# A convolution and two feed-forward layers on one core: the first tile's own tokens loaded apart, the tail's lower rows a step ahead, the last chunk in halves

## The reference

```python
w = exp(weight_gen - max); w /= sum + 1e-9        # [2, 4096, 8 heads, 7 taps]
x_pad = 6 zero tokens in front of each batch, then x    # [2, 4096, 192]
out[b, s, h, :] = sum over k of w[b, s, h, k] * x_pad[b, s + k, h, :]   # 24 channels a head
x = out.reshape(8192, 192)
x = (relu(x @ moe_w_in) ** 2) @ moe_w_out               # 192 -> 2048 -> 192
h = x @ moe2_w_in
out = (h * cos(h)) @ moe2_w_out                         # 192 -> 2048 -> 192
```

## Time and profile before

| | us |
|---|---|
| median of three executions | 1201.99 |
| the profiled execution | 1201.13 |
| its span in the profile | 1199.3 |
| TensorE busy | 1174.4 (98%) |
| VectorE busy | 963.7 (80%) |
| ScalarE busy | 816.2 (68%) |
| GpSimd busy | 369.3 (31%) |

### The profile page before, as it was taken

One profiled execution on the slowest core, in us unless ns is written; L12 is line 12 of the kernel. 1 busy time (PEld: TensorE's weight loads), 2 busy tenths in 40 slices (PEclk: granted clock), 3 DMA queues, 4 the chain that ended last, 5 costly groups with the idle time before them and its releaser, 6 DMA issues.

```text
span 1199.3 us, 25462 instructions
## 1 busy us (share of the span) xinstructions
PE 1174.4 (98%) x9784; PEld 1108.5 (92%) x9784; DVE 963.7 (80%) x1500; ACT 816.2 (68%) x1488; POOL 369.3 (31%) x265
## 2 busy tenths in 40 slices
PE   5999999999999999999999999999999999999997
PEld 4778999899999999999999999999999999999986
DVE  7867888877878787787878878787787878878786
ACT  3887666666666676666666666666666767666675
POOL 3895707052150704307060240705215070000000
PEclk9999999999999999999999999999999999999999
DMA  7432111011110111111011111101111000100000
GB/s 183 103 86 48 34 28 34 8 21 34 28 34 14 18 35 24 34 27 34 12 18 34 28 34 21 35 13 22 34 28 34 13 17 4 25 1 14 1 15 14
DMA packets 112984, 37.30 MB, mean 31 GB/s; under 512 B 101600, under 2 KB 110816, under 8 KB 112864
## 3 DMA queue, kind: packets, MB, share of 16 engines
q1 hardware_dynamic: 110974, 34.75, 13.9%
q10 hardware_dynamic: 1890, 0.93, 0.4%
HBM read 23.84 MB, written 6.29 MB: 25 GB/s over the span
## 4 chain that ended last, share of the span: by engine, by line
PE 87%; DVE 6%; ACT 4%; issue 1%; DMA 0%; SPq 0%; POOL 0%; ACTq 0%; DVEq 0%; POOLq 0%
PE y L557 45%; PE h L557 41%; DVE h L1237 1%; DVE h L1259 1%; DVE turns L1241 1%; ACT turns L1001 1%; DVE g_lo L1272 1%; ACT relu L974 1%; ACT g_hi L1014 1%; DMA xc<-in_x_dram 0%; DVE g_lo L1268 0%; DVE x L1227 0%; ACT arena L957 0%; DVE stat L1129 0%; DVE stat L1120 0%
## 5 line engine op out<-in xcount | busy, mean ns | idle before, releaser
L557 PE MATMUL y<-g_hi,wo 64*128 64x512 f32 x3054 | 703.6, 395 | 1.1 <-DVE g_lo L1163 0.5
L557 PE MATMUL y<-g_lo,wo 64*128 64x512 f32 x2036 | 528.3, 391 | 0.0
L557 PEld LDWEIGHTS y<-g_hi,wo 64*128 64x128 f32 x3054 | 425.2, 184 | 25.0 <-DVE xa_lo L1286 2.8
L478 POOL TENSOR_TENSOR tap<-xc,gen 128x768 f32<-128x768 f32 x98 | 150.9, 1546 | 581.6 <-DVE xd_lo L1249 566.1
L557 PEld LDWEIGHTS y<-g_lo,wo 64*128 64x128 f32 x2036 | 311.7, 184 | 5.1
L557 PE MATMUL h<-xa_hi,wa_hi 64*128 64x512 f32 x1018 | 278.5, 404 | 6.0 <-DVE g_lo L1268 4.1
L1001 ACT ACTIVATE turns<-turns 128x512 f32<-128x512 f32 x238 | 150.4, 632 | 196.8 <-DVE turns L1241 195.8
L557 PE MATMUL h<-xa_hi,wa_lo 64*128 64x512 f32 x1018 | 269.6, 391 | 0.0
L557 PE MATMUL h<-xa_lo,wa_hi 64*128 64x512 f32 x1018 | 269.0, 391 | 0.0
L1259 DVE TENSOR_TENSOR h<-h,turns 128x512 f32<-128x512 f32 x238 | 165.9, 697 | 122.6 <-ACT turns L1001 121.7
L1237 DVE SCALAR_TENSOR_TENSOR h<-h,relu 128x512 f32<-128x512 f32 x249 | 173.4, 696 | 66.9 <-ACT relu L974 64.3
(11 more groups left out here) (101 smaller groups left out, 1092.3 us busy)
## 6 DMA issues: line engine op xcount, KB each, us to landing
xc<-in_x_dram SPq DMA_DIRECT2D x60, 240.0 KB
out_dram<-arena SPq DMA_DIRECT2D x62, 64.0 KB, 1.9
xt_a<-x_blocks SPq DMA_DIRECT2D x224, 16.0 KB, 1.8
arena<-in_moe_w_out_dram SPq DMA_DIRECT2D x16, 192.0 KB, 3.4
arena<-in_moe_w_in_dram SPq DMA_DIRECT2D x16, 128.0 KB, 2.7
out_dram<-arena SPq DMA_DIRECT2D x62, 32.0 KB, 1.7
xt_d<-x_blocks SPq DMA_DIRECT2D x112, 16.0 KB, 1.8
arena<-in_moe_w_in_dram SPq DMA_DIRECT2D x16, 64.0 KB, 3.0
```

The lines of the kernel that those rows point to most:

```text
L478: pool.tensor_tensor(tap[:, k % 2, :].rearrange("p (r g) -> p r g", g=GROUP), rows[k], wk, ALU.mult).then_inc(pool_step, 1)
L557: return pe.matmul(o, w[rows, :], x[rows, :], start=start, stop=stop)
```

## The change

At the start, xc is filled by 11 transfers. `load_first_own` loads the four own rows of each partition in four transfers with a semaphore of their own, `x_own`; `load_first_halo` loads the six halo rows in seven. SP issues seven of the eleven, ScalarE four. The convolution takes the taps from the newest to the oldest: the first product waits for `x_own` only, the second for all. The last product is cut into heads 0 to 5 and heads 6 to 7, the last two sums into channels 0 to 127 and 128 to 191, and TensorE turns part 0 as soon as the first group of channels is complete. One group of eight identity transposes is gone.

In the tail, a slot starts with BOTTOM's first up matmul, ahead of the wait for g_lo, and with the previous chunk's `up_d_top`; BOTTOM's up matmuls are one step ahead of TOP's down matmuls through the slot. Chunk 255's columns go in two halves of 256 from engine to engine, with a bank of h each, and the last three chunks' down matmuls start with the three that need only g_hi, without waiting for g_lo.

```diff
-    FIRST_X = 16 * 8
+    FIRST_OWN = 16 * QUARTERS
+    FIRST_X = 16 * 7
@@ start of SP; ScalarE has the rest
-            load_first_rows(sp, ((0, 0), (0, 1), (0, B), (1, 0)))
+            load_first_own(sp, (0, 1))
+            load_first_halo(sp, ((1, B), (0, 0), (0, 1), (1, 0), (1, 1)))
@@
+        def parts(m):
+            count = 2 if m == STEPS - 1 else 1
+            return [(k, slice(k * TOK // count, (k + 1) * TOK // count)) for k in range(count)]
+        def load_first_own(eng, quarters):
+            for q in quarters:
+                eng.dma_start(xc[q * BLOCK:(q + 1) * BLOCK, HALO * DM:],
+                              x_v[:, q * JJ * DM:(q + 1) * JJ * DM]).then_inc(x_own, 16)
@@ TensorE: the last down matmuls
+            def last_down(k, y, l, f, hi, lo):
+                w = wo[l]
+                for part, cols in parts(k):
+                    part_a, part_d = y[:, 0, cols], y[:, 1, cols]
+                    pe.wait_ge(g2_hi_ready, k + 1 + part)
+                    pe.matmul(part_a, w[:, f, 0:DA], hi[:, cols], start=False, stop=False)
+                    pe.matmul(part_a, w[:, f, 2 * P:2 * DM], hi[:, cols], start=False, stop=False)
+                    pe.matmul(part_d, w[:, f, DA:2 * P], hi[:, cols], start=False, stop=False)
...
@@ TensorE: tail_slot
+                    if m == STEPS - 1:
+                        last_tail_up(m, k)
+                        return
+                    up_a(o, 1, f, of, BOTTOM, 0, start=True)
+                if STEPS - SLOTS < m < STEPS:
+                    end_of_tail_up(m - 1)
+                if m < STEPS:
+                    pe.wait_ge(g2_ready, k + 1)
...
-                for j in range(3):
-                    last = down_a(down, TOP, j, start=j == 0)
-                    up_a(o, 1, f, of, BOTTOM, j, start=j == 0)
-                last.then_inc(tail_a_left, 1)
-                pe.wait_ge(down2_done, k)
-
-                top = m >= STEPS - SLOTS
-                down_d(down, TOP, 0, start=True)
+                for j in range(2):
+                    up_a(o, 1, f, of, BOTTOM, j + 1)
+                    down_a(down, TOP, j, start=j == 0)
                 up_d(o, 1, f, of, 0)
-                down_d(down, TOP, 1).then_inc(tail_d_left, 1)
+                down_a(down, TOP, 2).then_inc(tail_a_left, 1)
                 if not top:
                     up_d(o, 1, f, of, 1)
                 up_d(o, 1, f, of, 2).then_inc(h2_left, 1)
+                pe.wait_ge(down2_done, k)
+                down_d(down, TOP, 0, start=True)
                 pe.wait_ge(tail_a_left, turn)
                 down_a(down, BOTTOM, 0)
+                down_d(down, TOP, 1).then_inc(tail_d_left, 1)
                 down_a(down, BOTTOM, 1)
+                down_a(down, BOTTOM, 2, stop=True).then_inc(tail_a_done, 1)
                 pe.wait_ge(h2_left, m)
                 up_a(o, 1, f, of, TOP, 0)
-                down_a(down, BOTTOM, 2, stop=True).then_inc(tail_a_done, 1)
-                up_a(o, 1, f, of, TOP, 1)
                 pe.wait_ge(tail_d_left, turn)
                 down_d(down, BOTTOM, 0)
+                up_a(o, 1, f, of, TOP, 1)
+                down_d(down, BOTTOM, 1, stop=True).then_inc(down2_done, 1)
                 last = up_a(o, 1, f, of, TOP, 2, stop=not top)
@@ TensorE: start
-            for k in range(TAPS - 1):
+            for k in range(TAPS - 2):
...
             pe.wait_ge(first_sum, TAPS - 1)
+            turn_x1(0, 0)
+            pe.wait_ge(first_sum, TAPS + 1)
             pe.wait_ge(pad_zeroed, 1)
-            for part in range(2):
-                turn_x1(0, part)
+            turn_x1(0, 1)
@@ ScalarE: tail_chunk (VectorE's in the same way)
                 if m < STEPS:
-                    act.wait_ge(up2_done, m + 1)
                     act.wait_ge(g2_made, m - 1)
-                    act.activation(turns[:, c, :], h[:, tail_bank(m), :], ACT.Copy,
-                                   bias=0.25).then_inc(turns_ready, 1)
+                    for part, cols in parts(m):
+                        act.wait_ge(up2_done, m + 1 + part)
+                        act.activation(turns[:, c, cols], h[:, tail_bank(m + part), cols], ACT.Copy,
+                                       bias=0.25).then_inc(turns_ready, 1)
```

More of the change, by code:

```diff
@@ L665, in downs_of_slot, with end_of_tail_up, last_tail_up @@
                         pe.wait_ge(piece_ready[PL + (m - D2) // PF], 3)
+            def end_of_tail_up(m):
+                f = m % SLOTS
+                if f % 4 == 0:
+                    pe.wait_ge(w_copied, f // 4 + 1)
+                    pe.wait_ge(x2_hi_ready, 2 * TILES + 1)
+                up_d_top(h[:, tail_bank(m), :], f, stop=True).then_inc(up2_done, 1)
+            def last_tail_up(m, k):
+                f, of = m % SLOTS, m // SLOTS % 2
+                (o, cols), (o2, cols2) = [(h[:, tail_bank(m + part), :], at) for part, at in parts(m)]
+                down = (y1, 1, k % SLOTS, g2_hi[:, k % 2, :], g2_lo[:, k % 2, :])
+                turn = k - (TAIL - LAG - TAIL_D2) + 1
+                up_a(o, 1, f, of, BOTTOM, 0, cols, start=True)
+                up_a(o, 1, f, of, BOTTOM, 1, cols)
+                end_of_tail_up(m - 1)
+                up_a(o, 1, f, of, BOTTOM, 2, cols)
+                up_d(o, 1, f, of, 0, cols)
+                pe.wait_ge(g2_ready, k + 1)
+                pe.wait_ge(tail_a_done, turn - 1)
+                down_a(down, TOP, 0)
+                up_d(o, 1, f, of, 2, cols).then_inc(h2_left, 1)
+                pe.wait_ge(g2_ready, m - 2)
+                up_a(o2, 1, f, of, BOTTOM, 0, cols2, start=True)
+                down_a(down, TOP, 1)
+                up_a(o2, 1, f, of, BOTTOM, 1, cols2)
+                up_a(o2, 1, f, of, BOTTOM, 2, cols2)
+                down_a(down, TOP, 2).then_inc(tail_a_left, 1)
+                up_d(o2, 1, f, of, 0, cols2)
+                up_d(o2, 1, f, of, 2, cols2).then_inc(h2_left, 1)
+                pe.wait_ge(down2_done, k)
+                down_d(down, TOP, 0)
+                pe.wait_ge(h2_left, m)
+                up_a(o, 1, f, of, TOP, 0, cols)
+                up_a(o, 1, f, of, TOP, 1, cols)
+                pe.wait_ge(tail_a_left, turn)
+                down_a(down, BOTTOM, 0)
+                up_a(o, 1, f, of, TOP, 2, cols)
+                up_d_top(o, f, cols, stop=True).then_inc(up2_done, 1)
+                down_a(down, BOTTOM, 1)
+                down_d(down, TOP, 1).then_inc(tail_d_left, 1)
+                down_a(down, BOTTOM, 2).then_inc(tail_a_done, 1)
+                pe.wait_ge(h2_left, m + 1)
+                up_a(o2, 1, f, of, TOP, 0, cols2)
+                up_a(o2, 1, f, of, TOP, 1, cols2)
+                pe.wait_ge(tail_d_left, turn)
+                down_d(down, BOTTOM, 0)
+                up_a(o2, 1, f, of, TOP, 2, cols2)
+                up_d_top(o2, f, cols2, stop=True).then_inc(up2_done, 1)
+                down_d(down, BOTTOM, 1).then_inc(down2_done, 1)
@@ L685, in tail_slot @@
                 if m >= STEPS:
-                    pe.wait_ge(down2_done, k)
-                    down_alone(*down).then_inc(down2_done, 1)
+                    if m == STEPS:
+                        pe.wait_ge(down2_done, k)
+                    last_down(k, *down)
                     return
@@ L716, in tail_slot @@
                     last.then_inc(up2_done, 1)
[L717 to L722, removed]
             def last_downs(m, o, f, of):
@@ L1208, in convolve_first @@
                 total = x1[:, 0:JJ * DM]
+                last = TAPS - 1
+                wide = -(-DA // GROUP)
                 def product(k):
@@ L1228, in convolve_first @@
                                       ALU.add).then_inc(first_sum, 1)
+                last_product(0, wide)
+                dve.wait_ge(first_product, last)
+                dve.wait_ge(first_sum, last - 2)
+                channel_sum(last - 1, 0, DA)
+                last_product(wide, HEADS)
+                dve.wait_ge(first_product, last + 1)
+                dve.wait_ge(first_sum, last - 1)
+                channel_sum(last, 0, DA)
+                channel_sum(last - 1, DA, DM)
+                dve.wait_ge(first_product, last + 2)
+                dve.wait_ge(first_sum, last + 1)
+                channel_sum(last, DA, DM)
             def slot(t, i, par):
```

107 lines of the change are left out of this document (70 added, 37 removed).

## The result

| | runs | us, median | range |
|---|---|---|---|
| before | 14 | 1201.67 | 1200.99 to 1203.00 |
| after | 14 | 1199.84 | 1197.63 to 1200.20 |

The ratio is 0.9981, 95% interval 0.9973 to 0.9988: 1.8 us faster where 4.0 were forecast. The time lies in the range, but the gain is under the 2.4 us from which the forecast called a kernel faster (0.73); it falls under "same", which had 0.21. The profiled execution took 1197.96 us (span 1196.1), 3.2 us less than that of before.

The account below looks back on a forecast made before the run. TensorE, busy 1174.4 of 1199.3 us, was taken to bound the kernel, so only its ends could gain: start 1.2, tail slots 1.1, last chunk 1.7, together 4.0 us from 1201.99 to 1198.0, range 1196.0 to 1200.3.

Parts of the forecast that it names:

- Clock, "charge nothing": Start, TensorE: with five warm-up groups the clock rises within the fifth group or by the turn; no cost charged.
- Rival C: Start: TensorE still at 1.2 GHz when real matmuls begin, rise at 32 us costing 6.2 us, 1204.2 us; chance 0.05.
- Tail slots, 1.1 us: Tail: slot period falls from 2.45 to 2.36 us, 8 slots giving 0.76; with the anchors 1.1 us, bounds -0.2 and 1.3.
- rival A: Tail: both array halves lock in step, the third y matmul's wait keeps the period at 2.45; 1198.8 us; chance 0.2.
- The two anchors: TensorE's waits for g_lo before slots 241 and 245: some 0.22 us gained, then 0.15 more until slot 247.
- Last chunk, 1.7: End of the tail: chunk 255 in two halves shortens the final chain from 10.17 to 8.45 us; gain 1.7, bounds 1.1 and 2.0.
- Loads, 1.4 at the second product: Start: first product at 7.2 needs only own tokens, second starts at 8.45, not 9.88; gain 1.4 us, bounds 0.6 and 1.8.
- start 2.3 for 1.2: Start: 1.6 us gained at the first chunk, 1.3 at operations behind it, 1.2 kept in the sum; bounds 0 and 1.7.
- tail 2.05 for 2.8: Tail: the forecast gains of 1.1 us in slots and anchors and 1.7 us in the last chunk.

Follow-up runs that it names:

- e9: The kernel after, unchanged, run again on another occasion beside others on one chip: 1199.78 us, three of eight runs at 1197.82 to 1197.99, five at 1199.77 to 1200.09.
- e1: The new start alone, with the loop and tail of the kernel before: 1199.96 us over 11 runs, in two groups, 1199.62 to 1199.96 and 1201.81 to 1202.53.
- e6: The kernel after with the sixth transpose group back and the upper half's third y matmul ahead of the lower half's first d-part up matmul: 1197.57 us.
- e8: The kernel before with five of its six groups of identity transposes, nothing else changed: 1204.51 us, ratio to before 1.0019.
- e2: The new tail slots and last chunk in halves, with the start and six warm-up groups of the kernel before: 1199.95 us over 11 runs.
- e7: The kernel after with the sixth transpose group back and the last chunk at its full width of 512 tokens: 1199.16 us over 11 runs.
- e10: The kernel after with the sixth transpose group back ahead of the turns, on e9's chip: 1198.01 us, one of seven runs at 1200.22.

## Why the prediction was right, and where not

*Clock, "charge nothing": failed.* The text weighed when the clock rises, and that came as said (0.86 us in the last group, or sooner: e9, the same kernel, has its fourth group at 1.11 us). It did not ask what happens after the rise. With the group ahead of the turns gone, TensorE idles, and in most executions the clock falls back to 1.2 GHz with the first chunk, at a price of 2.0 to 2.2 us (the trace of e1; the two groups of runs in after, e1 and e9). Rival C had the place and the missing group, at a chance of 0.05, but another mechanism: a late rise, with a price that grows by 1.5 us per slot. Its 1.4 us per early chunk fits (e1's second relu comes 3.15 us after the first and not 1.79); the growth doesn't, since in e1 nothing lasting is added behind the second chunk. The rows contradicted the Trainium skill on transposes ("TensorE: Matmul & The Clock Gate", Part 4), and they still do: nothing but identity transposes had run when the loads went from 1.56 to 0.86 us. But all of this is on the rise, and the rise is not what failed.

*Tail slots, 1.1 us: failed, by the wait that rival A named, for another reason.* "The upper half must lead by 0.1; it can": it does lead (1177.53 against 1177.61), and that does not help. The count that the lower half waits for came with the end of the h matmul ahead of it in the program. The period was 2.425; with that one order changed 2.38, near the forecast's 2.36. Shown by rows: in after the load follows the h matmul, in e6, with the two swapped, the y matmul, at a fixed distance each time; and the swap gives 0.49 us over the tail. So a matmul counted as done here only when the one ahead of it in the program was done too. From the tail's first turns to those of chunk 254 after takes 39.19 us (1145.49 to 1184.68), the profiled execution of before 39.34, e8's 39.37 and e1's 39.55: the slots gave 0.15 to 0.36 us. The two anchors, 0.37 in the sum, gave nothing that shows: up to the turns of chunk 246 after takes 19.79 us and before 19.71, and the eight slots behind it bring 0.23 of the 0.76. (The rule of the Trainium skill named with rival A, same page, Part 3, has matmuls both start and end in program order. The starts don't follow it: the y matmul at 1177.53 stands behind the h matmul at 1177.61 in the program. The counts that the waits see do.)

*Last chunk, 1.7: right in the size, partly by luck.* 1.64 measured. The chain gave 1.36, of which the new order alone accounts for 0.57. Its parts were a little off: counted from the start of chunk 254's turns, those of the two halves come at 1.89 (forecast 2.17 - 0.19 = 1.98), the last g_lo ends at 5.74 (5.64), but the matmuls behind it take 0.72 where 0.51 was counted; the stores' 0.28 made most of that good, and were not in the sum.

*Loads, 1.4 at the second product: right, 1.65 in the profiled pair.* It started at 8.23 for 8.45. The first product came at 6.78, not 7.2, because ScalarE's queue issues less and its exponentials end earlier. Against the median the start is worth more, 2.3 us (1.95 by the spans). The old first product waited for the whole load, whose end varies: it started at 9.01, 9.20 and 9.99 in the profiles of before, e2 and e8. The new second product started between 7.66 and 8.38 in eleven. The executions show the same: the spans of e2's 11, with the old start, spread over 1.8 us, those of e7's 11, with the new one, over 0.4. The prediction took the loads of before's profiled execution as typical, and that execution lies 0.86 us under its median.

*The sum.* At full clock after takes 1197.8, which is the forecast's 1198.0, but by two errors that cancel: start 2.3 for 1.2, tail 2.05 for 2.8. The clock then takes 2.1 us in some two thirds of the executions (15 of 22 in after and e9). That the median, 1199.84, is still in the range is luck: nothing in the sum stands for this loss, and rival C, the one that names the clock, forecast 1204.2, outside the range.

## What to carry to other kernels

When a change starts real work on TensorE earlier, move the filler work with it, up to the first real matmul, and compare the mean granted clock of many executions: one profile can show the good case. In this kernel a wait on a matmul was a wait on what stands ahead of it in the program too, so let the matmul that counts go first. One profiled execution is a sample of the loads' luck; a stage that waits for a load gains in its spread as well as in its mean.

## What the runs showed of the hardware that was not expected

The granted clock fell back from 2.4 to 1.2 GHz in some executions of one and the same program and not in others: in e1 just before 21 us, in e8 before 22, in e10 after 22, with the turns or the first real matmuls already running. In e1 it stayed down until after 27.5 us, in e8 until after 31.5, with TensorE busy in nearly all of that time. The rise before it moves as well. The first group of eight loads that takes less than 1.5 us is the fifth in after (at 16.19), the fourth in e9, the same kernel (at 14.60), and the second in e8 (at 13.61, 1.42 us). Why one execution of after in three escapes is open.
